# An expert's first layer as a product of 512 columns, its halves added by ScalarE and VectorE

## The reference

```python
def _moe2_ref(x, modality_id, w_gate, modality_bias, w1, w2):
    logits = x @ w_gate + modality_bias[modality_id]
    e_idx = np.argmax(logits, axis=1)
    ...
    for e in range(E):                       # E = 8
        mask = e_idx == e
        h = np.maximum(x[mask] @ w1[e], 0.0) # w1[e]: 512 x 1024
        out[mask] = gate_w[mask, None] * (h @ w2[e])   # w2[e]: 1024 x 512
```

## Time and profile before

| | us |
|---|---|
| median of 3 runs | 882.04 (881.56 to 885.13) |
| the profiled execution | 881.52 |
| its span, first to last instruction | 879.8 |
| TensorE busy | 864.5 (98%) |
| VectorE busy | 623.3 (71%) |
| ScalarE busy | 381.6 (43%) |
| GpSimd busy | 178.3 (20%) |

### The profile page before, as it was taken

One profiled execution on the slowest core, in us unless ns is written; L12 is line 12 of the kernel. 1 busy time (PEld: TensorE's weight loads), 2 busy tenths in 40 slices (PEclk: granted clock), 3 DMA queues, 4 the chain that ended last, 5 costly groups with the idle time before them and its releaser, 6 DMA issues.

```text
span 879.8 us, 22177 instructions
## 1 busy us (share of the span) xinstructions
PE 864.5 (98%) x7992; PEld 810.2 (92%) x7992; DVE 623.3 (71%) x1482; ACT 381.6 (43%) x925; POOL 178.3 (20%) x289
## 2 busy tenths in 40 slices
PE   7999999999999999999999999999999999999996
PEld 5788999999999999999999999999999999999994
DVE  6766876875876875875876873348877777777774
ACT  4556534333333343343442442243455555555555
POOL 2352212222212222212222221101100000000001
PEclk9999999999999999999999999999999999999999
DMA  8735623123123123033123021152561113511111
GB/s 232 211 121 161 225 61 97 48 84 103 32 85 109 47 86 108 26 91 104 56 82 92 30 81 61 37 193 61 160 225 48 48 48 108 178 48 48 48 49 37
DMA packets 94296, 82.86 MB, mean 94 GB/s; under 512 B 51070, under 2 KB 74112, under 8 KB 94208
## 3 DMA queue, kind: packets, MB, share of 16 engines
q1 hardware_dynamic: 89728, 68.02, 26.4%
q0 software_dynamic: 4192, 13.66, 4.2%
q10 hardware_dynamic: 288, 0.00, 0.0%
HBM read 56.18 MB, written 25.54 MB: 93 GB/s over the span
## 4 chain that ended last, share of the span: by engine, by line
PE 97%; DMA 1%; ACT 1%; DVE 0%; issue 0%; POOLq 0%; SPq 0%; ACTq 0%
PE acc_a L344 7%; PE acc_b L344 7%; PE acc_a L346 6%; PE acc_b L346 6%; PE acc_a L345 6%; PE acc_b L345 6%; PE misc L340 4%; PE misc L338 4%; PE misc L339 4%; PE s_even L1006 3%; PE acc_a L338 3%; PE acc_b L338 3%; PE acc_b L340 3%; PE acc_b L339 3%; PE attn L339 2%; PE attn L340 2%
## 5 line engine op out<-in xcount | busy, mean ns | idle before, releaser
L866 POOL TENSOR_TENSOR probs<-scores,row_inv 128x256 f32<-128x256 f32 x96 | 67.2, 720 | 278.3 <-DVE row_inv L1975 278.3
L1448 ACT ACTIVATE ew<-raw_e 128x1024 fp32r (+1 forms) x92 | 93.1, 1050 | 12.0 <-issue 10.9
L344 PE MATMUL acc_a<-xT_w,w 128*128 128x384 f32 x256 | 89.4, 349 | 0.0
L344 PE MATMUL acc_b<-xT_w,w 128*128 128x384 f32 x256 | 87.9, 343 | 0.0
L346 PE MATMUL acc_a<-xT_w,w 128*128 128x384 f32 x256 | 86.6, 338 | 0.0
L346 PE MATMUL acc_b<-xT_w,w 128*128 128x384 f32 x256 | 86.5, 338 | 0.0
L345 PE MATMUL acc_a<-xT_w,w 128*128 128x384 f32 x256 | 86.5, 338 | 0.0
L345 PE MATMUL acc_b<-xT_w,w 128*128 128x384 f32 x256 | 86.5, 338 | 0.0
L1474 ACT ACTIVATE scores<-scores,neg_max 128x136 f32<-128x136 f32 x192 | 75.9, 397 | 20.6 <-DVE neg_max L1965 20.6
L1448 ACT ACTIVATE uT_w<-ab 128x384 fp32r<-128x384 f32 x64 | 33.3, 520 | 92.5 <-DVE ab L2027 92.5
L942 POOL DMA_INDIRECT out<-row_out,ids_i x24 | 25.6, 1065 | 222.5 <-DVE row_out L2144 212.1
(11 more groups left out here) (393 smaller groups left out, 2911.2 us busy)
## 6 DMA issues: line engine op xcount, KB each, us to landing
raw_e<-in_moe_w SPq DMA_DIRECT2D x24, 512.0 KB, 7.9
raw<-in_moe_w SPq DMA_DIRECT2D x16, 512.0 KB, 6.2
x_in<-routed SPq DMA_DIRECT2D x100, 64.0 KB, 2.1
v_nat<-in_v SPq DMA_DIRECT2D x24, 256.0 KB, 3.0
x_mid<-x_out SPq DMA_DIRECT2D x24, 256.0 KB, 2.0
x_in<-x_mid SPq DMA_DIRECT2D x24, 256.0 KB, 2.8
q_nat<-in_q SPq DMA_DIRECT2D x80, 64.0 KB, 2.3
k_nat<-in_k SPq DMA_DIRECT2D x80, 64.0 KB, 2.0
```

What stands on the lines that cost most here:

```text
L344: pe.matmul(o, w_hi, x_hi, start=start, stop=False, skip_group_check=True)
L866: pool.tensor_tensor(probs[:, at, side * HALF:(side + 1) * HALF], scores[:, at, side, SINKS:], row_inv[:, at].unsqueeze(2).broadcast_to([P ...
L1448: return act.activation(o, i, ACT.Copy)
```

## The change

For the pairs from unit 2 on the first layer is computed in another way. The high weights are multiplied with the high and the low rows in one matmul of 512 columns: its moving operand is `uT_w[:, :, c, 0:256]`, two pieces of 256 columns that lie apart, and its output is the whole PSUM bank. A second matmul adds low weights times high rows to the first half. ScalarE copies the second half to SBUF (`h_part`), VectorE adds the first half to it (`h_sum`), ScalarE takes the ReLU of the sum from SBUF, and VectorE the difference from it. Units 0 and 1 keep `unit_h`, and the few rows are as before.

The semaphores `h_copied` and `h_summed` are two that the stage before has left at 16 (`w3T_hi`, `w3T_lo`). The waits of TensorE move with the work: a bank is free when the sum of four blocks back is done, and the second layer of the first tile waits for four, six and eight differences before chunks 0, 4 and 6. On VectorE the order changes as well: the difference of block k - 1 stands behind the sum of block k, both transposes stand behind the last difference, and both scalings stand behind the x differences of the next unit.

```diff
@@ TensorE
+            def pair_h(u, k):
+                o = h_banks[k % 4]
+                pe.wait_ge(h_summed, h_pieces(u, k - 3) if k >= 4 else h_pieces(u, 0))
+                if k == 0:
+                    for tile in range(2):
+                        pe.wait_ge(X_lo[tile], u + 1)
+                for c in range(KD):
+                    if k == 0:
+                        pe.wait_ge(e1_lo, splits_before(u) + c + 1)
+                    pe.matmul(o[:, :].rearrange("p (a n) -> p a n", a=2), ew1_hi[:, c, k * P:(k + 1) * P],
+                              uT_w[:, :, c, 0:EXPERT_ROWS], start=c == 0, stop=False, skip_group_check=True)
+                    mm = pe.matmul(o[:, 0:EXPERT_ROWS], ew1_lo[:, c, k * P:(k + 1) * P], xT_hi[:, c, :],
+                                   start=False, stop=c == KD - 1, skip_group_check=True)
+                mm.then_inc(h_full, 1)
...
+            def pair_y(u, tile):
...
+                for c in range(KF):
+                    if tile == 0 and c in (0, 4, 6):
+                        pe.wait_ge(h_lo, 8 * u + H_BEFORE + {0: 4, 4: 6, 6: 8}[c])
@@ ScalarE, pair(u)
                 for k in range(KF):
-                    unit_h(u, 2, k)
+                    act.wait_ge(h_full, 8 * u + k + 1)
+                    copy(h_part[:, k % 2, :], h_banks[k % 4][:, EXPERT_ROWS:2 * EXPERT_ROWS]).then_inc(h_copied, 1)
...
                     if k < KD:
                         unit_w2(u, need, buf, k)
+                    act.wait_ge(h_summed, h_pieces(u, k + 1))
+                    act.activation(uT_hi[:, k, :], h_sum[:, k % 2, :], ACT.Relu).then_inc(h_hi, 1)
@@ VectorE
+            def pair_sum(u, k):
+                ve.wait_ge(h_copied, h_pieces(u, k + 1))
+                ve.wait_ge(h_lo, 8 * u + (H_BEFORE + k - 1))
+                ve.tensor_tensor(h_sum[:, k % 2, :], h_banks[k % 4][:, 0:EXPERT_ROWS], h_part[:, k % 2, :], ALU.add).then_inc(h_summed, 1)
+            def pair_lo(u, k):
+                ve.wait_ge(h_hi, 8 * u + k + 1)
+                ve.scalar_tensor_tensor(out=uT_lo[:, k, :], in0=h_sum[:, k % 2, :], scalar=0.0,
+                                        in1=uT_hi[:, k, :].bitcast(F32), op0=ALU.max, op1=ALU.subtract).then_inc(h_lo, 1)
             def pair(u):
                 buf = buf_of(u)
                 for k in range(KF):
-                    unit_h(u, 2, k)
+                    pair_sum(u, k)
+                    if k >= 1:
+                        pair_lo(u, k - 1)
                     if k < KD:
                         unit_w2(u, buf, k)
-                    if k >= KF - 2:
-                        turn_x(u + 1, k - (KF - 2))
-                turn(u, buf_of(u + 1))
+                pair_lo(u, KF - 1)
+                for tile in range(2):
+                    turn_x(u + 1, tile)
+                buf = buf_of(u + 1)
+                for c in range(KD):
+                    unit_w1(u + 1, buf, c)
+                unit_x(u + 1, 0)
+                unit_x(u + 1, 1)
+                unit_y(u, 0)
+                unit_y(u, 1)
+                next_gates(u, 2)
```

More of the change, by code:

```diff
@@ L145, in build @@
             few_rows = sb("few_rows", [P, 2, 2 * P], F32, last)
+            h_part = sb("h_part", [P, 2, EXPERT_ROWS], F32, last)
+            h_sum = sb("h_sum", [P, 2, EXPERT_ROWS], F32, last)
         raw8 = sb("raw8", [P, 8, WIDE * 2])
@@ L269, in build @@
         expert_in = w1_in + w3_in[0:KD]
+        h_copied, h_summed = w3T_hi, w3T_lo
         split_hi = sem("split_hi")
@@ L356, in slots_in, with h_pieces @@
             return 16 + 5 * 16 * u
+        def h_pieces(u, k):
+            return 2 * F // P - 2 * 8 + 8 * u + k
         def few_slots_in(n_pairs, u):
@@ L1211, in unit_h @@
                 mm.then_inc(h_full, 1)
+            def pair_h(u, k):
[13 more added lines that the diff above has]
+            def pair_y(u, tile):
+                o, at = y_banks[tile], slice(tile * P, (tile + 1) * P)
+                pe.wait_ge(y_done[tile], u)
+                if tile == 0:
+                    pe.wait_ge(e2_lo, splits_before(u) + KD)
+                for c in range(KF):
+                    if tile == 0 and c in (0, 4, 6):
+                        pe.wait_ge(h_lo, 8 * u + H_BEFORE + {0: 4, 4: 6, 6: 8}[c])
+                    mm = triple(pe, o[:, :], uT_hi[:, c, at], uT_lo[:, c, at], ew2_hi[:, c, :], ew2_lo[:, c, :], c == 0, c == KF - 1)
+                mm.then_inc(y_full[tile], 1)
             def unit_y(u, tile, chunks=range(KF)):
@@ L1399, in pair @@
                 for k in range(KF):
-                    unit_h(u, 2, k)
-                unit_y(u, 0)
-                unit_y(u, 1)
+                    pair_h(u, k)
+                pair_y(u, 0)
+                pair_y(u, 1)
             def few(u):
@@ L1429, in few @@
                 mm.then_inc(y_full[0], 1)
-            pair(1)
+            for k in range(KF):
+                unit_h(1, 2, k)
+            unit_y(1, 0)
+            unit_y(1, 1)
             pe.wait_ge(known, JOBS_KNOWN)
@@ L2464, in buf_of @@
                 return ve.value_load(buf_i[0:1, bass.ds(u, 1)], min_val=0, max_val=1)
[L2466 to L2473, removed]
             ve.wait_ge(known, WEIGHTS)
```

## The result

The changed kernel takes 889.70 us (median of 5 runs, 889.50 to 889.83) against 882.37 for the kernel before in the same comparison: ratio 1.0079, 95% interval 1.0062 to 1.0095. The forecast was 887.2 and slower, with a range of 880 to 893: the time is in the range, 2.5 above the forecast. The profiled execution has a span of 888.0 us, 8.2 over the 879.8 of before.

What follows compares the result with a forecast made beforehand. TensorE bound the kernel, 22.44 us a pair; VectorE with ScalarE would take over at 22.72. Start +1.1, eight cycles +2.2, small product in all +5.2: 886.7 from 881.5, 887.2 against the median; range 880 to 893.

Steps and rivals of the forecast that it cites:

- The mechanism: In the pairs, VectorE with ScalarE becomes the clock at 22.72 us, above TensorE's 22.01; chance 0.5.
- The signs: In the trace: TensorE waits 0.5 to 1 us before first layers, units 22.7 apart, sums 1.25 apart in blocks 4 to 7.
- The cycle: One pair walked along VectorE: 19.88 + 0.72 + 1.01 + 1.11 = 22.72 us, against 22.44 before.
- The start: TensorE's first layer of unit 3 starts at 666.16 instead of 665.05: +1.1 us.
- The end: Behind the last pair, ScalarE takes the few rows' small product at 874.5, before at 869.31: +5.2 us.
- what follows keeps its distances: After ScalarE takes the small product, the rest of the kernel was to keep its spacing, adding nothing to +5.2.
- TensorE's saving: First layer: 0.0135 us for each of 32 products, 0.43 us a pair, 4.3 over ten; not in the sum.
- the two bounds: TensorE's gain: 0 if the two-piece operand pays the fixed 0.0135 us twice, 4.3 us if not.
- three hand-offs: Between VectorE and ScalarE: each 0.06 us off a hand-off is worth 1.8 us, counting three times in nine cycles.
- It can't shorten the cycle: Moving both scalings behind the x differences spares 0.72 us before TensorE's wait, but was said not to shorten the cycle.
- The first rival: Hand-offs and small instructions are cheaper, so the chain fits under TensorE's 22.01 us: about 879.5 us; chance 0.15.

Runs made afterwards that it cites:

- the halves apart: Against the kernel before: only TensorE's matmuls changed, 879.00 us; changed kernel with the 512-column product as two of 256, 890.56 us.
- the extra sums: Changed kernel plus three unused 256-column sums on VectorE per pair: in blocks 1 to 3 898.47 us, in blocks 5 to 7 888.14 us.
- the copies ahead: Changed kernel, but from block 3 on ScalarE copies the half of block k + 1 before the ReLU of block k: 881.90 us.
- one edit more: Changed kernel with ScalarE copying the half of block k + 1 before the ReLU of block k, from block 3 on: 881.90 us.
- with two: Changed kernel with ScalarE copying a block ahead from block 3 on, and the last unit's small product after one weight copy, not two: 880.09 us.
- the late sums: Changed kernel plus three unused 256-column sums on VectorE, in blocks 5, 6 and 7 of each pair: 888.14 us.
- the transposes: Changed kernel with VectorE's two transposes back in blocks 6 and 7: 893.75 us.
- TensorE's half alone: Kernel before with only TensorE's 512-column and low products; ScalarE and VectorE unchanged, reading the first half of the bank only: 879.00 us.
- loads ahead with the transposes: Changed kernel with transposes back in blocks 6 and 7 and ScalarE's two register loads ahead of the last ReLU's wait: 890.33 us.
- the early extra sums: Changed kernel plus three unused 256-column sums on VectorE, in blocks 1, 2 and 3 of each pair: 898.47 us.

## Why the prediction was right, and where it was off

- **The mechanism** was right: the chain copy, sum, ReLU, difference on two engines sets the pace in TensorE's place. It is shown by the halves apart, the extra sums and, above all, the copies ahead. The signs came as forecast too: sums 1.27 apart (1.25), a wait before each first layer of up to 0.8 us (0.5 to 1), ScalarE not idle before the small product. The unit starts are 22.9 apart (22.7), and the products of 512 columns 0.24 from their successors (0.2265).
- **The cycle** was forecast at 22.72 and is 22.88, over eight cycles 22.92 on average. From the first sum to the end of the x differences it is 19.75 (19.88 forecast; the weight difference of block 1 hardly waited, the alternation took 1.27 and not 1.25). What was too small lies behind: second tile to gate copy 1.13, not 1.01, and gate copy to first sum 1.28, not 1.11. Both were read where VectorE had just waited for TensorE; here its queue was full of work, and the sum waits on more register values. Which of these it is was not tried.
- **The start** was forecast at +1.1 for unit 3 and is +1.6: the first sum at 646.56, not 646.20, and x difference to TensorE 0.32, not 0.08. That hand-off had been taken without a row.
- **The end** was forecast at +5.2 and is +6.9 at the small product: the start is 0.5 more, the eight cycles 1.6 more (+3.8, not +2.2) and ScalarE's queue 0.4 less. The sentence "what follows keeps its distances" failed: +1.3 for the lower clock. In the profiled executions the forecast was +5.2 and the result is +8.2. The medians are only 2.5 from the forecast, because 0.5 had been added to it for the kernel before, and the changed kernel's profiled execution was no quicker than its median.
- **TensorE's saving** was 0.32 and not 0.43 a pair, between the two bounds. Whether the two pieces of the operand cost the rest, or the alternation of 512 and 256 columns, is not shown: no run had a product of 512 columns in one piece there. It mattered nothing here.
- **Two small slips in its sums**: 0.06 off three hand-offs in nine cycles is 1.6 us (1.8 needs the last pair as a tenth), and ScalarE's 384 columns are recorded at 0.52 in the earlier trace rows, not 0.53. Neither moves the forecast.
- **"It can't shorten the cycle"**, of VectorE's order, was right for the order as changed and wrong as a rule: the old order costs 0.67 a cycle.
- **The first rival** (the chain fits, about 879.5) came true with one edit more, at 881.9, and at 880.1 with two.

## What to carry to other kernels

When an engine with 5 us of spare time a cycle gets 2.5 us more work, ask how many hand-offs the work adds in series: here two engines that alternate needed 1.27 us a block for 0.68 us of work, and issuing the first step of the next block before the last step of this one brought that to 0.79, and the pair back to what TensorE needs. Idle time in such an alternation is free for work nobody waits for, as the late sums show, and not for work that holds up the next link, as the transposes show. A cycle has several loops of nearly one length, so look for the second before shortening the first.

## What the runs showed of the hardware

- The moving operand in two pieces: a product of 512 columns and one of 256 take 0.351 us together, 0.0045 more than the sum of the spacings that the earlier trace rows give (0.2265 and 0.120).
- VectorE needs 0.42 recorded, 0.34 start to start, for 256 fp32 columns, whether it reads one operand from PSUM or both from SBUF.
- TensorE's granted clock was 1.00 in each stretch of 20 us from 440 to 860 in the changed kernel, and 0.50 from 877.5 to 880.5, after a wait of 1.5 us at 875 to 876.6. Over the profiled executions it goes with that wait, but not always. With 0.6 to 0.7 us of wait the 64 products took 1.95 to 2.13 us (kernel before, TensorE's half alone, loads ahead with the transposes). With 1.5 to 2.5 us they took 2.62 to 3.46 in seven executions, and 1.95 in one, the late extra sums. So one execution's profile can't say whether this 1.3 us belongs to a kernel. In the late extra sums the mean granted clock of each run goes with its time (0.998 at 888, 0.996 at 890), and the changed kernel has 0.996 five times, which suggests that it pays the 1.3 us each time; with the early extra sums the runs have 0.995 to 0.998 and the same time within 0.2, so this isn't shown.
- Two register loads behind a wait cost ScalarE 1.1 us of idle time, and none where they could be issued ahead of it.
